# Turning the recurrent state on VectorE instead of ScalarE, with the mask, joins and maxima reordered, in a chunked complex linear attention followed by two feed-forward stages

## The reference, cut to what matters

```python
B, H, S, D = 4, 8, 768, 48
mag = np.sqrt(a_re * a_re + a_im * a_im)
scale = np.minimum(mag, 0.999) / (mag + 1e-06)
a_re_n, a_im_n = (a_re * scale, a_im * scale)
for t in range(S):
    new_re = ar * S_re - ai * S_im          # ar, ai: a_re_n, a_im_n at t
    new_im = ar * S_im + ai * S_re
    S_re, S_im = (new_re + k[t] (x) v[t], new_im)
    y[:, :, t] = q[:, :, t] @ S_re
x = y as (3072, 384)
h = max(max(x @ w1, x @ w2), x @ w3)        # 384 -> 768
x2 = h @ w_out                              # 768 -> 384
# then a router picks one of 8 experts for each row of x2:
# out = gate * (relu(x2 @ w1[e]) @ w2[e])   # 384 -> 1024 -> 384
```

## Time and profile before

| | us |
|---|---|
| median of 3 runs | 907.98 |
| lowest and highest | 906.64, 908.34 |
| the profiled execution | 906.64 |
| its span | 904.9 |
| PE, PEld busy | 798.0 (88%), 740.6 (82%) |
| DVE, ACT, POOL busy | 641.8 (71%), 483.0 (53%), 508.3 (56%) |

### The profile page before, as it was taken

The page is one execution under the profiler, slowest core; times in us unless marked ns, Lnnn a source line. Parts: engine busy times, 40 slices in busy tenths (PEclk is TensorE's granted clock), DMA queues, the critical chain, the costliest instruction groups (busy, mean ns, idle before and its releaser), DMA issues.

```text
span 904.9 us, 18765 instructions
## 1 busy us (share of the span) xinstructions
PE 798.0 (88%) x6641; PEld 740.6 (82%) x6642; DVE 641.8 (71%) x1046; ACT 483.0 (53%) x977; POOL 508.3 (56%) x873
## 2 busy tenths in 40 slices
PE   0567898988988999999999999949999999999995
PEld 0435887878878888888899999938999999997894
DVE  5989789899797989899887755277332353547821
ACT  5685857776766767776545654234211242436611
POOL 1199989799999999999985000003323333234322
PEclk9769899999999999999999999977999999999998
DMA  9401152453424242423311110445511142417211
GB/s 305 130 11 43 32 146 76 117 132 96 116 76 110 77 111 93 112 76 84 86 51 56 56 41 22 159 150 184 192 35 49 50 153 79 154 59 269 97 36 45
DMA packets 41876, 89.74 MB, mean 99 GB/s; under 512 B 6264, under 2 KB 23680, under 8 KB 40480
## 3 DMA queue, kind: packets, MB, share of 16 engines
q1 hardware_dynamic: 37632, 76.04, 27.7%
q0 software_dynamic: 4160, 12.60, 4.2%
HBM read 69.74 MB, written 17.69 MB: 97 GB/s over the span
## 4 chain that ended last, share of the span: by engine, by line
PE 51%; POOL 17%; DVE 17%; issue 7%; ACT 4%; DMA 2%; ACTq 0%; DVEq 0%; SPq 0%; POOLq 0%
POOL c_im L2102 5%; POOL c_re L2101 4%; PE yu L1731 4%; PE yu L1735 4%; PE yu L1732 4%; POOL ring L2105 4%; PE mm L1731 4%; POOL ring L2104 4%; PE mm L1735 3%; PE mm L1732 3%; PE tr L2003 2%; PE mm L2004 2%; PE tr L2004 2%; PE mm L2003 2%; PE mm L2005 2%
## 5 line engine op out<-in xcount | busy, mean ns | idle before, releaser
L1731 PE MATMUL mm<-up_hi,x_hi 128*128 128x384 f32 x432 | 156.4, 362 | 3.0 <-DVE h_sb L1194 2.6
L1732 PE MATMUL mm<-up_lo,x_hi 128*128 128x384 f32 x432 | 147.5, 341 | 0.0
L2101 POOL TENSOR_TENSOR c_re<-ring 112x128 f32<-112x128 f32 x165 | 106.0, 642 | 58.0 <-DVE ring L1147 36.4
L2178 POOL DMA_INDIRECT out_rows<-g_o,rows_out x30 | 35.3, 1176 | 145.4 <-DVE g_o L1583 132.4
L2102 POOL TENSOR_TENSOR c_im<-ring 112x128 f32<-112x128 f32 x165 | 114.4, 693 | 0.0
L1735 PE MATMUL mm<-up_hi,x_lo 128*128 128x384 f32 x432 | 99.8, 339 | 1.2 <-DVE x_lo L1182 1.2
L2105 POOL TENSOR_TENSOR ring<-c_re,c_im 112x64 f32<-112x64 f32 x165 | 97.0, 588 | 0.0
L2104 POOL TENSOR_TENSOR ring<-c_re,c_im 112x64 f32<-112x64 f32 x165 | 88.0, 533 | 12.9
L2154 POOL DMA_INDIRECT g_in<-x_scratch,rows_in x34 | 37.9, 1114 | 94.1 <-DVE rows_in L1546 69.0
L1731 PEld LDWEIGHTS mm<-up_hi,x_hi 128*128 128x128 f32 x432 | 82.5, 191 | 8.2 <-issue 4.3
L1194 DVE TENSOR_TENSOR h_sb<-mm,h_sb 128x384 f32<-128x384 f32 x96 | 52.8, 550 | 44.0 <-PE mm L1735 43.8
(11 more groups left out here) (261 smaller groups left out, 2242.7 us busy)
## 6 DMA issues: line engine op xcount, KB each, us to landing
raw<-in_moe_w SPq DMA_DIRECT2D x16, 1536.0 KB, 9.1
a_dn<-in_a_laid SPq DMA_DIRECT2D x18, 384.0 KB, 7.1
an_scratch<-a_dn SPq DMA_DIRECT2D x18, 384.0 KB, 2.3
ring<-an_scratch SPq DMA_DIRECT2D x18, 384.0 KB, 5.6
q_in<-in_q_laid SPq DMA_DIRECT2D x24, 224.0 KB, 2.8
k_in<-in_k_laid SPq DMA_DIRECT2D x24, 224.0 KB, 3.1
v_in<-in_v_laid SPq DMA_DIRECT2D x24, 192.0 KB, 3.2
x_scratch<-x_sb SPq DMA_DIRECT2D x24, 192.0 KB, 2.0
```

What stands on the lines that cost most here:

```text
L1731: nc.tensor.matmul(out, hi[:, x, :], w_hi(x), start=(x == 0), stop=False)
L1732: nc.tensor.matmul(out, hi[:, x, :], w_lo(x), start=False, stop=False)
L2101: nc.gpsimd.tensor_tensor(c_re[:, 0:count, :, :], cur, bc(prev[:, :, 0, :], 2, 2), ALU.mult).then_inc(chain_prod, 1)
```

## The change

1. The products of the rotation leave ACT. DVE makes them with two `tensor_tensor` of 384 elements, the turn broadcast along the innermost 48. The turn's table `rot` grows to four planes, the last one negated, so that one addition of 384 replaces an addition and a subtraction of 192. POOL writes the plane twice in one instruction, and has one more instruction (`none - r`) with a wait ahead of it; one more memset stands in its setup.
2. `mask(n)` moves ahead of `moe_h_lo(n-2, 1)` in all rounds but 1, 3 and 5.
3. The early joins, outside `late_z` rounds, all stand behind `moe_max(n-1, 0, 1)` and ahead of `add_state`; before, the first stood ahead of that maximum and a second one behind `moe_max(n-1, 0, 2)`.
4. `maxima_first(n)` holds only for n < 9. From round 9 the order is late join, `norm_inverse`, third maximum. `moe_h_lo(n-1, 0)` is now last in every round. ACT's `norm_rest` of rounds 9 and later stands at the end of its own round, ahead of the next `moe_x_hi`.

```diff
@@ (setup, and maxima_first)
+        none = sb1("none", [R, PER, HP])
-        rot = sb1("rot", [R, NC, 2, HP])
+        rot = sb1("rot", [R, NC, 2, 2, HP])
...
-            return n in joins_late
+            return n in joins_late and n < 9
@@ (scalar)
-            def rotation(n):
-                if n % CB == 0:
-                    return
-                act.wait_ge(rot_ready, 2 * (n // PER + 1))
-                act.wait_ge(x_ready, n)
-                for y, (dst, src) in enumerate(((st_same, st_x[:, :, :, :]), (st_other, st_x[:, ::-1, :, :]))):
-                    for h in range(HP):
-                        last = nc.scalar.activation(dst[:, :, h, :], src[:, :, h, :], ACT.Copy, scale=rot[:, n, y, h:h + 1])
-                    last.then_inc(turned, 1)
...
-                if now and 1 <= n < 6:
-                    rotation(n)
...
-                if more and n >= 5:
-                    rotation(n + 1)
@@ (vector)
+                turn = [bc(rot[:, n, y, :, :], 3, D) for y in range(2)]
+                dve.wait_ge(rot_ready, 3 * (n // PER + 1))
+                dve.wait_ge(x_ready, n)
+                nc.vector.tensor_tensor(flat(st_same[:, :, :, :]).rearrange("p (y d) -> p y d", d=D), flat(st_x[:, :, :, :]).rearrange("p (y d) -> p y d", d=D),
+                                        turn[0].rearrange("p x h d -> p (x h) d"), ALU.mult).then_inc(turned, 1)
+                nc.vector.tensor_tensor(st_other[:, :, :, :], st_x[:, ::-1, :, :], turn[1], ALU.mult).then_inc(turned, 1)
                 dve.wait_ge(turned, 2 * (n - n // CB))
                 wait(dve, y_done, n)
-                for x, op in ((0, ALU.add), (1, ALU.subtract)):
-                    nc.vector.tensor_tensor(flat(st_t[:, x, :, :]), flat(st_same[:, x, :, :]), flat(st_other[:, x, :, :]), op).then_inc(t_ready, 1)
+                nc.vector.tensor_tensor(flat(st_t[:, :, :, :]), flat(st_same[:, :, :, :]), flat(st_other[:, :, :, :]), ALU.add).then_inc(t_ready, 1)
...
+                if now and not late_z:
+                    mask(n)
                 if prev2:
                     moe_h_lo(n - 2, 1)
...
-                if now:
+                if now and late_z:
                     mask(n)
...
-                for g, number in early[:1] if not late_z else ():
-                    join(g, number)
                 if prev:
                     moe_max(n - 1, 0, 1)
+                for g, number in early if not late_z else ():
+                    join(g, number)
...
-                for g, number in early[1:] if not late_z else ():
-                    join(g, number)
...
                 if maxima_first(n):
                     moe_max(n - 1, 1, 1)
-                    moe_h_lo(n - 1, 0)
...
                 if prev and not maxima_first(n):
                     moe_max(n - 1, 1, 1)
+                if prev:
                     moe_h_lo(n - 1, 0)
@@ (gpsimd)
+            link(nc.gpsimd.memset(none[:, :, :], 0.0))
...
-                nc.gpsimd.tensor_tensor(r[:, :, 0, :], rp[:, 0, :, 0, :], rp[:, 1, :, 1, :], ALU.subtract).then_inc(rot_ready, 1)
-                nc.gpsimd.tensor_tensor(r[:, :, 1, :], rp[:, 0, :, 1, :], rp[:, 1, :, 0, :], ALU.add).then_inc(rot_ready, 1)
+                nc.gpsimd.tensor_tensor(r[:, :, 0, :, :], bc(rp[:, 0, :, 0, :], 2, 2), bc(rp[:, 1, :, 1, :], 2, 2), ALU.subtract) \
+                    .then_inc(rot_ready, 1)
+                nc.gpsimd.tensor_tensor(r[:, :, 1, 0, :], rp[:, 0, :, 1, :], rp[:, 1, :, 0, :], ALU.add).then_inc(rot_ready, 1)
+                pool.wait_ge(rot_ready, 3 * g + 2)
+                nc.gpsimd.tensor_tensor(r[:, :, 1, 1, :], none[:, :, :], r[:, :, 1, 0, :], ALU.subtract).then_inc(rot_ready, 1)
```

More of the change, by code:

```diff
@@ L1224, in add_state @@
                 else:
-                    dve.wait_ge(t_ready, 2 * (n - n // CB))
+                    dve.wait_ge(t_ready, n - n // CB)
                     nc.vector.tensor_tensor(dst, yu[0:R, 1, 0:2 * YW].rearrange("p (x w) -> p x w", x=2), st_t[:, :, :, :].rearrange("p x h d -> p x (h d)"), ALU.add) \
@@ L1820, in answers @@
                 if not alone:
-                    pe.wait_ge(t_ready, 2 * (n - n // CB))
+                    pe.wait_ge(t_ready, n - n // CB)
                     for both in ((0, 1), (3, 2)):
@@ L2118, in turns @@
                 pool.wait_ge(rp_ready, 2 * (g + 1))
-                r = rot[:, g * PER:(g + 1) * PER, :, :]
-                nc.gpsimd.tensor_tensor(r[:, :, 0, :], rp[:, 0, :, 0, :], rp[:, 1, :, 1, :], ALU.subtract).then_inc(rot_ready, 1)
-                nc.gpsimd.tensor_tensor(r[:, :, 1, :], rp[:, 0, :, 1, :], rp[:, 1, :, 0, :], ALU.add).then_inc(rot_ready, 1)
+                r = rot[:, g * PER:(g + 1) * PER, :, :, :]
+                nc.gpsimd.tensor_tensor(r[:, :, 0, :, :], bc(rp[:, 0, :, 0, :], 2, 2), bc(rp[:, 1, :, 1, :], 2, 2), ALU.subtract) \
[3 more added lines that the diff above has]
+                nc.gpsimd.tensor_tensor(r[:, :, 1, 1, :], none[:, :, :], r[:, :, 1, 0, :], ALU.subtract).then_inc(rot_ready, 1)
             chain_steps(1, range(1, 11))
```

## The result

The changed kernel takes **923.27 us** (median of 4 runs, 922.94 to 923.33) where the kernel before takes 908.16 (median of 4, 906.64 to 909.38): a ratio of 1.0167, interval 1.0149 to 1.0184. It is 1.7% slower. Its profiled execution took 924.32 us with a span of 922.5; that of before was 906.64 and 904.9. Round n is again counted from opening maximum to opening maximum on DVE.

What follows compares the result with a forecast made beforehand. PE and DVE, waiting on each other, were taken to bound rounds 10 to 17, POOL those up to 9. 906.64 + 9.1 (rounds 10 to 17) + 1.4 (round 18 on) + 2.9 (rounds 1 to 9) = 920.0 us; range 909 to 926.

Steps and rivals of the forecast that it cites:

- Even rounds: Rounds 10 to 17: first maximum waits for PE, join follows; +1.43 us each, about +2.5 in round 12.
- That the rotation costs nothing in rounds 10 to 17: DVE's extra 1.2 us of rotation per round fills its idle time ahead of the first maximum, at no cost.
- Odd rounds: Rounds 10 to 17: the mask ahead delays h_lo and so PE; +0.73 us per odd round.
- The length of a round for PE: Round 19, 19.5 us with PE always busy, taken as PE's own length; round 15 has 1.7 us of waits.
- The signs: PE waits about 1.3 us for h_lo at L1776; norm_rest waits under 2.6; g = 6 join 2 to 4 later.
- Round 18: The early join again precedes the second maximum, for which product group 4 waits: +1.4 us, bounds 0 and 2.66.
- POOL's terms: From the g = 4 chain to the g = 6 join: three turns +0.9 us, five rotations slowing POOL +2.0.
- The term for what now stands behind the join of g = 6: Third maximum and h_lo, 0.94 us, move behind that join, having been done in its wait before: +0.9 us.
- Rounds 1 and 2: Round 1 gains up to 2.1 us on ACT, round 2 loses 1.2 to the mask; g = 4 load 0.9 earlier.
- Faster: Rival: PE's two waits go and nothing replaces them; 898 to 900 us, chance 0.12.
- POOL sets the pace: Rival: blocking is whole, POOL's chains grow 3 us or more each, late rounds wait for joins; over 926 us, chance 0.08.
- The rotation is what costs: Rival: products over 0.8 us each overrun DVE's idle time; 922 to 926 us, part of the main case, no separate chance.

Runs made afterwards that it cites:

- the late order alone: Kernel before; from round 9 late join and norm_inverse precede the third maximum, norm_rest precedes x_hi; h_lo behind every late join: 909.44 us, ratio 1.0004.
- The turns alone: Kernel before with only POOL's larger turn table and its one more instruction and wait per g; ACT still rotates: 909.26 us, ratio 1.0016.
- The products alone: Kernel before with DVE making the two rotation products as well, while ACT keeps its rotation and POOL its table: 914.49 us, ratio 1.0074.
- late order from round 11: Kernel before; late join and norm_inverse ahead of third maximum, norm_rest early, only from round 11; h_lo behind every late join: 908.32 us, ratio 1.0001.

## Why the prediction was right, and where it was not

**Direction and size.** I forecast 920.0 us within 909 to 926, slower with 0.82; it is 923.27. Of the 3.3 us between, 1.5 are the distance of the profiled execution of before (906.64) to the median (908.16), which the prediction left out of its sum. The rest is the sum itself, 13.4 us against a difference of medians of 15.1. That they lie so close is in part luck: terms that were wrong by up to 4.8 us stand in it with opposite signs. By the table it was 3.7 us too low up to round 10 and 0.8 too high in rounds 10 to 17; the profiled execution of the changed kernel lies 1.05 us above the median, so these lines add up to more than the medians do.

**Even rounds: right in mechanism and size, but for round 10.** I counted a first maximum 8.33 us in, a second 13.99 in, and 22.80 for the round. Round 14 has 8.27, 13.94 and 22.65; round 12, for which the same path was claimed, has 8.33, 13.89 and 22.80. The joins alone give what the same path gives without the mask's delay: 7.60 + 2.66 + 3.00 = 13.26 for the second maximum, where the trace has 13.28, and +0.64 for the round; with the mask ahead as well the changed kernel has +1.27. In round 14 DVE still idles 0.50 us ahead of the first maximum, so the rotation's products fit into the hole that the moved join leaves.

Round 10 is the exception. Its +1.66 is near the term of 1.43, but undoing the mask or the joins leaves it at 22.66 and 22.41 us, undoing both leaves 22.98, and the late order alone makes it 22.87 and the rotation alone 22.11, from 20.98. The joins alone make it only 21.69. So the right size is luck there: what the late order brings, `h_lo` behind a join that waits for POOL, and then the slow clock, was not in the prediction.

**That the rotation costs nothing in rounds 10 to 17: wrong in the old order, not measured in the new.** In odd rounds it holds but for one (round 13 with the rotation alone, 21.65 us in place of 21.18). But added alone on DVE, in the old order, it makes rounds 14 and 16 1.2 and 1.4 us longer, since DVE had no gap there. In rounds 10 to 17 the parts alone cost 4.4 (mask), 3.3 (joins), 2.9 (rotation) and 0.2 us (late order), 10.8 in sum, and together 8.3. Each of the first three alone lengthens rounds 10, 14 and 16, of 21.0 to 21.4 us, to between 21.7 and 22.1, and all together make them 22.6 to 23.0: there they do not add up. The 0.2 of the late order is a sum of a loss of 1.9 in round 10 and of gains behind it. What the rotation costs inside the changed kernel was not measured: the changed kernel with the rotation back on ACT was not run. On top of the late order it costs 2.5 us in these rounds, nearly all of it in rounds 13, 14 and 16.

**Odd rounds: right in mechanism, too large in two of three.** The term was +0.73. Round 11 has +0.85, rounds 13 and 15 +0.18 and +0.15. The step that failed is the start of the mask. I took the time from the opening maximum to the mask as it was, 3.45 us; in round 15 it is 2.90 (412.52 to 415.42), as `x_lo` and the two instructions on `n_m` are shorter: 0.54, 0.56 and 0.58 us, where the same three took 0.74, 0.81 and 0.67. `h_lo` thus starts 4.10 in and not 4.64, and PE goes on 4.70 in, 0.19 behind the old 4.51. In round 11 the mask starts 3.26 in, PE goes on 5.05 in, and there the price is near what I counted. The mask alone shows the same: it starts 3.40, 3.40 and 2.91 in in rounds 11, 13 and 15, and these pay 0.87, 0.59 and 0.17. Why these instructions are shorter in one round than in another is open.

**The length of a round for PE: misread.** The window 477.60 to 497.10 was taken for round 19. By opening maxima round 19 runs from 480.27 to 498.70, 18.43 us, and rounds 18 to 23 take 17.9 to 20.5 us each, so that no single length stands for PE's own round, and the 1.7 us of waits read from the difference is not shown; the two waits in round 15 are 1.42 us. The window of round 12 began 4 us early too, but its length, 20.10, is near the 20.17 between the maxima. The sum did not rest on the 19.5.

**The signs.** PE's wait ahead of the last three matmuls in the second half of `moe_down` was said to be about 1.3 us; it is 0.35 to 1.10 in rounds 11 to 17, and the wait in the first half, 0.58 to 1.42, was not foreseen. PE no longer waits for `h_hi`, as said. `norm_rest` was to wait less than 2.6 us; it waits 3.9 to 4.8, as ACT comes to it sooner, without the rotation and with `x_hi` behind it. It does start 0.93 us earlier against the opening maximum, as counted. The join of g = 6 starts 5.7 us later than 290.85 and not 2 to 4; 3.9 of it is the late start of the chain of g = 4.

**Round 18: right.** +1.6 in the round, +1.4 over rounds 18 and 19, and the joins undone give it back.

**POOL's terms: right one by one, not together.** The turns alone lengthen the stretch from the chain of g = 4 to the join of g = 6 by 0.9 us, as counted; but in the four kernels with mask, joins or late order alone, in which neither turns nor rotation change, it is between as long as before and 0.9 us shorter, so 0.9 is hardly clear of the spread. The products alone lengthen it by 2.1, for a term of 2.0. The sizes do not hold in every order: with the rotation alone the stretch grows by 4.1, and in the changed kernel by only 1.8. The rule of the Trainium skill ("SBUF — State Buffer", "Who interferes with whom"), by which all of the added DVE time could fall on POOL, would have given 6. Over the eight chains of g = 2 to 9 the products alone cost POOL 10.5 us for 13 rotations, 15.6 us of DVE work at my 1.2 us each: two thirds of it, and not all. The term for what now stands behind the join of g = 6 was right too (+0.9).

**Rounds 1 and 2: wrong.** The step was "the load for g = 4 is thus about 0.9 us earlier"; it is 3.9 us later. Two things failed in it. In round 1 the gain on ACT was counted as up to 2.1 us. From DVE's join behind the wait at 50 us to round 2 the kernels with the rotation on DVE alone take 57.2 to 58.9 us (the changed kernel 58.9 in both traces) and the others 59.5 to 60.9: a gain there is, but in the changed kernel it is only 0.7 us, and round 2 begins at 110.3 where it began at 110.52. With the mask back and with the joins undone it begins at 109.2, and up to there PE, DVE and ACT run the same list as in the changed kernel. So this difference is not one of the order, and its cause is open. A late load of `x_raw` does not settle it: `x_hi` starts at 85.4 and 85.7 us in the changed kernel, but at 87.67 with the rotation alone, where round 2 begins at 109.6. In round 2 I priced the mask at its own length, 1.2 us, as if PE had lost only the wait. That holds where the clock stays at 1.00 (+1.07 with the mask alone). Here the wait became 2.88 us, and the clock fell behind it: 3.8 us in the round. Little of that reaches the end: undoing it brings 2.6 us at round 10, 1.7 at round 20, and 0.4 in the median. That POOL and the loads, for which rounds 3 to 13 also wait, take up the rest is likely and not shown.

**The rivals.** *Faster* decided on whether `h_lo` ends within 4.5 us of the opening maximum: it ends 4.64 us in in round 15 (416.62 + 0.54, from 412.52). What it said of PE's old waits was true in that they went; others came in their place. *POOL sets the pace* was not the case of the changed kernel, but it is that of the rotation alone and of the mask undone, where rounds are short enough for POOL to be late. *The rotation is what costs* has 923.27 in its range of 922 to 926, but not its reason: DVE still idles ahead of the first maximum in round 14 (0.50 us) and in round 15 (0.55).

## What to carry to other kernels

An engine that is relieved of work gains only where its result is what others wait for last; before moving work, ask what the receiving engine has to hand on at that time, and put nothing in front of that, not even an instruction of 1.2 us that is late anyway. Price an order by the start of the one instruction that the bottleneck waits for, and do not add up the prices of edits that lengthen the same stretch. An instruction that a third engine needs does not belong behind one that may wait for a fourth, as `h_lo` behind a join that waits for POOL.

## What the runs showed of the hardware

A wait of PE can cost more than its length. After waits of 2.88 and 2.90 us in round 2 the granted clock was 0.50 in one window of 3 us and 0.54 and 0.60 in the next. After waits of 4.01 and 4.00 us in round 10 (both traces of the changed kernel) it was 0.54 and 0.50 from 301 to 304 us, and after 3.86 us (late order from round 11) 0.50. In round 6 of the changed kernel, where two joins now stand between the first maximum and the second, PE waits 4.03 us and the clock is 0.50 from 223 to 226; with the joins alone it falls at this place too. The length of the wait does not decide alone. After 2.84 us with the mask alone and 2.61 with the joins undone, in round 2, and after 2.55 in round 10 of the kernel before, the clock stayed at 1.00. With rotation and late order it fell to 0.68 and 0.75 where PE had waited 1.69 us, and in the kernel before it is 0.62 from 187 to 190 us, where PE waits 1.80 us. The Trainium skill ("TensorE: Matmul & The Clock Gate", "Part 1: The HAM clock gate") says that the clock is set by how busy PE has recently been, and that it has two levels. The rows of 0.50 and 1.00 agree with the levels. What tells the waits with a fall from those without is open here.

DVE instructions of one form are not of one length: `x_lo` took 0.54 us in one round and 0.74 in another. Where POOL was idle beside it (rounds 20, 22, 23 and 24 in both traces) it took 0.54 to 0.56; the long ones all have a busy POOL beside them, but so have many short ones. Sums made of the durations of a single round carry an error of some half a microsecond over five instructions, as large as the effect that was at stake in the odd rounds.
